# Leaky activation of a fused attention, MLP and switch-MoE kernel: slope and bend on ScalarE, and the rounding handed from GpSimd to ScalarE two tiles later

## Chip, cores and metric

One core of one Trainium2 chip runs the whole program. The time is device microseconds of one execution; for each kernel the median of several executions is taken. The profile is of one further execution.

## What is computed

Top-32 attention (4 batches, 8 heads, 576 tokens, width 64), then an MLP with a leaky activation, then a mixture of 8 experts. The change touches the second:

```
x = attention output as 2304 rows of 512
h = x @ w_in                                  # 512 -> 2048
g = maximum(h, 0) + alpha * minimum(h, 0)     # alpha: one value for each of the 2048 columns
x2 = g @ w_out                                # 2048 -> 512, all float32
```

## The kernel before

**Attention.** There are 16 passes. A pass takes four heads and half of the 576 query rows, as nine tiles of 128 rows, in three groups of three tiles; group 0, 1 and 2 below. For each group VectorE searches the 32nd largest score of every row (`search`: MAX8 at L1050 and MATCH_REPLACE8 at L1063 in four rounds), then masks and sums the exponentials (L1070). The reciprocal of the sums (`invert`: L1079 and L1082) is computed inside the search of the following group, after its first two MAX8. GpSimd multiplies the three tiles by it (`normalise`, L1324), TensorE transposes them (L560, L561), ScalarE copies the transposes out (L856, L857), and TensorE multiplies by v (L571). ScalarE also copies the scores (L835) and computes the exponentials (L841, L844). Pass p+1's scores for groups 0 and 1 are made between the transposes of pass p.

**MLP.** A step is two passes, an even and an odd one. There are 8 steps; in steps 1 to 7 the 288 tokens of the step before also go through the MLP, and the last 288 go through it in a tail behind the last step. x, w_in, w_out and g are each split into a high and a low float16 part, and each product is three float16 matmuls. During the even pass TensorE makes h for 16 tiles f of 128 columns (L590, `up`), between transposes and score matmuls; during the odd pass it makes x2 (L604, `down`). `up` has two PSUM banks: tile f waits until ScalarE has read tile f-2. `down` waits for all 16 tiles of g (`g_ready`).

**The leak, for each tile f.** ScalarE, in `mlp_part`: Relu with scale s to `pos_part` (L882), Relu with scale -s to `neg_part` (L883), and, after waiting for its own semaphore, `neg_part` times -alpha (L886). Then `leak` on GpSimd: the sum (L358), the float16 high part (L360, a TENSOR_SCALAR), and sum minus high part (L362, the low part), each waiting for the one before. In the tail VectorE runs the same `leak`. `pos_part` and `neg_part` have four buffers; ScalarE's tile f waits until the low part of tile f-4 is done.

**Order on each engine.** Each engine works through a written order, and nothing overtakes. GpSimd in the even pass of steps 1 to 7: normalise group 0, two `low_x` subtractions, leak of tiles 0 to 4; normalise group 1, leak of tiles 5 to 11; normalise group 2, leak of tiles 12 to 15; then normalise group 0 of the odd pass. ScalarE in the even pass: for group 0 and then group 1, and for each of the three tiles j: copy the transposes, one or two leak tiles, copy a score tile, one or two leak tiles; with j = 0 it ends with the exponentials of the next group. So tiles 0 and 1 stand before the exponentials of group 1, tiles 8 and 9 before those of group 2, and tiles 14 and 15 are the last thing in the even pass. The odd pass begins on TensorE and ScalarE with group 2's transposes (the tiles of the even pass), score matmuls between them, and the products with v.

**Weights.** In step 0, without an MLP, ScalarE scales each of eight chunks of 2048 columns (four of w_in, then four of w_out) in place (L932) and rounds it (L936), and GpSimd subtracts (`split`). VectorE works out the scales in `close_weights` and `scale_weights` with small linked instructions between its searches.

```
leak_parts = {(0, 0): range(0, 5), (0, 1): range(5, 12), (0, 2): range(12, FT1)}
normalise(2 * i + par, par, g)
if g == 0:
    low_x(2 * i + par - 1)
leak(pool, nc.gpsimd, i - MLP_LAG, leak_parts.get((par, g), ()))
```

## Time and profile before

| | before |
|---|---|
| median of 3 runs | 1118.12 us (1116.74 to 1120.65) |
| profiled execution | 1123.2 us, span 1121.4 us |
| busy: TensorE, VectorE | 927.9 us (83%), 903.8 us (81%) |
| busy: ScalarE, GpSimd | 631.4 us (56%), 427.4 us (38%) |
| mean granted TensorE clock | 0.934 of full speed |

In the profile PE is TensorE's matmuls and PEld its weight loads, DVE is VectorE, ACT ScalarE, POOL GpSimd. L358 is line 358 of the kernel before. Times are microseconds from the start of the span unless marked ns. Behind an instruction, square brackets give how long its engine sat idle before it and who ended that.

### The profile page before, as it was taken

How to read it: one execution, taken by the hardware profiler on the slowest of the kernel's cores; microseconds unless marked ns; L12 is line 12 of the kernel's file. 1: busy time of each engine (PE TensorE's matmuls, PEld its weight loads, DVE VectorE, ACT ScalarE, POOL GpSimd, SP SyncE). 2: the span in 40 equal slices, each digit the busy share in tenths (PEclk: the TensorE clock that was granted, in tenths of full speed). 3: DMA queues.
4: the chain of work that ended last, by engine and by line, in shares of the span. 5: the costliest groups of instructions: out<-in, count | busy, mean ns of one | idle time of the engine just before them, and what ended most of it. 6: DMA issues, size and time to landing. Idle time of an engine off the chain costs nothing.

```text
span 1121.4 us, 22533 instructions
## 1 busy us (share of the span) xinstructions
PE 927.9 (83%) x6271; PEld 616.9 (55%) x6272; DVE 903.8 (81%) x1984; ACT 631.4 (56%) x1324; POOL 427.4 (38%) x598
## 2 busy tenths in 40 slices
PE   5346588898899889888988898899888889498996
PEld 2223256675666657665766575667556567243342
DVE  4999989999999999999999999999999270611110
ACT  3786969647855785587459637954883281010100
POOL 0136738514830682267028513840582100201110
PEclk9956589999999999999999999999999799699999
DMA  7910110013002200310031004001100166626650
GB/s 205 365 37 22 32 34 22 23 41 87 0 21 70 57 0 21 96 32 21 1 97 30 21 8 119 1 21 53 44 2 1 55 226 213 221 90 225 199 165 18
DMA packets 98658, 84.05 MB, mean 75 GB/s; under 512 B 69116, under 2 KB 77308, under 8 KB 98048
## 3 DMA queue, kind: packets, MB, share of 16 engines
q1 hardware_dynamic: 94544, 78.56, 23.0%
q0 software_dynamic: 1488, 3.15, 0.8%
q10 hardware_dynamic: 2528, 1.18, 0.4%
q8 instruction: 43, 0.70, 0.3%
q14 instruction: 55, 0.45, 0.1%
HBM read 72.64 MB, written 11.53 MB: 75 GB/s over the span
## 4 chain that ended last, share of the span: by engine, by line
PE 62%; POOL 12%; issue 11%; ACT 8%; DVE 4%; DMA 2%; POOLq 1%; ACTq 0%; DVEq 0%
PE acc L604 16%; PE acc L571 8%; PE sc L542 7%; PE pt_full L560 6%; PE acc L590 5%; POOL pos_part L358 5%; PE sc L712 3%; PE pt_full L772 3%; POOL arena L360 3%; POOL arena L1324 2%; PE pt_full L780 2%; PE sc L721 2%; PE acc L613 2%; ACT arena L844 1%; PE acc L619 1%
## 5 line engine op out<-in xcount | busy, mean ns | idle before, releaser
L1050 DVE MAX8 best<-arena 128x8 f32<-128x576 f32 x576 | 403.5, 742 | 9.8 <-ACT arena L835 6.6
L1063 DVE MATCH_REPLACE8 arena<-best,arena 128x576 f32<-128x576 f32 x432 | 315.8, 738 | 0.0
L1324 POOL TENSOR_SCALAR arena<-arena,row_inv 128x576 f32<-128x576 f32 x144 | 106.5, 757 | 351.3 <-DVE row_inv L1082 351.3
L590 PE MATMUL acc<-arena 128*128 (+1 forms) x1536 | 202.4, 286 | 28.0 <-ACT neg_part L883 26.1
L604 PE MATMUL acc<-arena 128*128 128x288 f16 x1536 | 202.2, 289 | 2.9 <-issue 2.9
L590 PEld LDWEIGHTS acc<-arena 128*128 128x128 f16 x1536 | 146.4, 98 | 78.8 <-issue 38.9
L604 PEld LDWEIGHTS acc<-arena 128*128 128x128 f16 x1536 | 149.6, 99 | 49.6 <-issue 12.9
L560 PE MATMUL pt_full<-ident,arena 128*128 128x128 f32 x576 | 102.4, 306 | 60.0 <-POOL arena L1324 34.4
L835 ACT ACTIVATE arena<-sc 128x576 f32<-128x576 f32 x144 | 92.1, 642 | 87.1 <-PE sc L542 70.6
L1070 DVE SCALAR_TENSOR_TENSOR arena<-arena,best 128x576 f32<-128x576 f32 x144 | 126.7, 927 | 5.9 <-ACT arena L844 5.9
L560 PEld LDWEIGHTS pt_full<-ident,arena 128*128 128x128 f32 x576 | 73.1, 155 | 90.3 <-POOL arena L1324 42.9
L542 PE MATMUL sc<-kT,qT 64*128 64x288 f32 x512 | 113.0, 478 | 7.0 <-ACT arena L835 5.0
L358 POOL TENSOR_TENSOR pos_part<-pos_part,neg_part 128x288 f32<-128x288 f32 x112 | 96.6, 863 | 48.6 <-ACT neg_part L886 48.6
L571 PE MATMUL acc<-arena,nat 128*64 128x288 f32 (+1 forms) x640 | 92.9, 431 | 20.4 <-ACT arena L857 13.7
L844 ACT ACTIVATE arena<-arena,neg_max 128x576 f32<-128x576 f32 x144 | 101.2, 765 | 1.6
L856 ACT ACTIVATE arena<-pt_full 128x512 f32<-128x512 f32 x128 | 75.5, 590 | 44.3 <-PE pt_rest L561 42.3
L362 POOL TENSOR_TENSOR arena<-pos_part,arena 128x288 f16<-128x288 f32 x112 | 86.7, 774 | 16.7 <-POOL arena L360 1.1
L542 PEld LDWEIGHTS sc<-kT,qT 64*128 64x128 f32 x512 | 63.1, 210 | 39.3 <-issue 20.1
L571 PEld LDWEIGHTS acc<-arena,nat 128*64 128x64 f32 (+1 forms) x640 | 45.0, 141 | 65.0 <-issue 49.8
L882 ACT ACTIVATE pos_part<-acc,scale 128x288 f32<-128x288 f32 x128 | 63.4, 495 | 26.6 <-PE acc L590 25.8
L886 ACT ACTIVATE neg_part<-neg_part,neg_alpha 128x288 f32<-128x288 f32 x128 | 68.5, 535 | 4.2
L883 ACT ACTIVATE neg_part<-acc,neg_scale_g 128x288 f32<-128x288 f32 x128 | 63.1, 493 | 0.0
(172 smaller groups left out, 942.2 us busy)
## 6 DMA issues: line engine op xcount, KB each, us to landing
arena<-in_moe_w_dram SPq DMA_DIRECT2D x64, 512.0 KB, 4.2
nat<-in_v_dram SPq DMA_DIRECT2D x64, 128.0 KB, 2.2
nat<-in_k_dram SPq DMA_DIRECT2D x60, 128.0 KB, 2.8
x_rows<-x2n SPq DMA_DIRECT2D x24, 192.0 KB, 2.4
out_dram<-x2n SPq DMA_DIRECT2D x24, 192.0 KB, 2.6
nat<-in_q_dram SPq DMA_DIRECT2D x64, 64.0 KB, 2.1
arena<-in_moe_w_in_dram SPq DMA_DIRECT2D x4, 1024.0 KB, 7.4
arena<-in_moe_w_out_dram SPq DMA_DIRECT2D x4, 1024.0 KB, 14.5
```

What stands on the lines that cost most here:

```text
L358: unit.tensor_tensor(pos, pos, neg, ALU.add).then_inc(leak_ready, 1)
L542: last = nc.tensor.matmul(dst[:, c, 0:HALF], qT[at, h // 2, r * P:(r + 1) * P], kT[at, h // 2, c * HALF:(c + 1) * HALF], start=True, stop= ...
L560: nc.tensor.transpose(pt_full[:, kt, :], src[:, kt * P:(kt + 1) * P], ident[:, :])
L571: last = nc.tensor.matmul(dst[h * D:(h + 1) * D, 0:HALF], v_nat[0:rows, par, 2 * c + h, kt, :], probsT[0:rows, 2 * c + h, kt, :], start=(k ...
L590: last = nc.tensor.matmul(dst[:, 0:HALF], win16[:, a, d, f * P:(f + 1) * P], xT16[:, bass.ds(row + d, 1), b, :].rearrange("p b s -> p (b s)"),
L604: last = nc.tensor.matmul(items.open[:, 0:HALF], wout16[:, a, f // (FT1 // OUT_CHUNKS), f % (FT1 // OUT_CHUNKS) * DM + d * P:f % (FT1 // O ...
L835: nc.scalar.activation(scores[:, t, :].rearrange("p (c s) -> p c s", c=2), sc[(TILES * par + t) % 2][:, :, 0:HALF], ACT.Copy).then_inc(s_s ...
L844: nc.scalar.activation(probs[:, gp, j, :], scores[:, GROUP * g + j, :], ACT.Exp, bias=neg_max[:, gp, j:j + 1], scale=SCALE).then_inc(exp_r ...
L1050: nc.vector.max(best[:, gp, j, r, :], src).then_inc(max_found if r == 0 else dve_step, 1)
L1063: nc.vector.match_replace(left[:, j, :], best[:, gp, j, r, :], src, MASKED).then_inc(dve_step, 1)
L1070: nc.vector.scalar_tensor_tensor(out=probs[:, gp, j, :], in0=tiles[j], scalar=best[:, gp, j, ROUNDS - 1, 7:8], in1=probs[:, gp, j, :], op0 ...
L1324: nc.gpsimd.tensor_scalar(probs[:, gp, j, :], probs[:, gp, j, :], row_inv[:, gp, j:j + 1], 1.0, ALU.mult, ALU.mult)\
```

## The change

ScalarE now reads h out of PSUM twice and no more: Copy with a scale `slope`, and Relu with a scale `bend`, both with one value for each column. slope is s times the smaller of alpha and 1, bend is s times (1 - alpha), and for alpha above 1 both signs are turned round by a `sign` that is also multiplied into w_out. GpSimd adds the two (`leak_sum`, waiting for `acc_stored`). The float16 high part is no longer GpSimd's: ScalarE rounds the sum of tile f-2 behind its two instructions for tile f (`round_leak`), and behind tile 15 the sums of 13, 14 and 15. GpSimd takes the low part of tile f-2 behind the sum of tile f (`leak_low`), and the last three behind sum 15. In the tail (the last 288 tokens) VectorE still adds, rounds and subtracts. In step 0 the scaling of a w_out chunk becomes four instructions of 512 columns instead of one of 2048, and VectorE has eight small instructions more and two less. No DMA is added, removed or moved.

```
-                        nc.scalar.activation(pos_part[:, f % NEG, :], src[:, 0:HALF], ACT.Relu, scale=scale[:, 3:4])
-                        nc.scalar.activation(neg_part[:, f % NEG, :], src[:, 0:HALF], ACT.Relu, scale=neg_scale_g[:, 0:1])\
+                        nc.scalar.activation(pos_part[:, f % NEG, :], src[:, 0:HALF], ACT.Copy, scale=slope[:, f:f + 1])
+                        nc.scalar.activation(neg_part[:, f % NEG, :], src[:, 0:HALF], ACT.Relu, scale=bend[:, f:f + 1])\
                             .then_inc(acc_stored, 1)
-                        act.wait_ge(acc_stored, items.base + items.used)
-                        nc.scalar.activation(neg_part[:, f % NEG, :], neg_part[:, f % NEG, :], ACT.Copy, scale=neg_alpha[:, f:f + 1])\
-                            .then_inc(parts_ready, 1)
+                        if not (isinstance(m, int) and m == HALVES - 1):
+                            for whole in range(f - 2, f - 1 if f < FT1 - 1 else FT1):
+                                if whole >= 0:
+                                    round_leak(m, whole)
...
+            def round_leak(m, f):
+                act.wait_ge(leak_summed, FT1 * m + f + 1)
+                nc.scalar.activation(gT16[0][:, f, :], pos_part[:, f % NEG, :], ACT.Copy).then_inc(leak_rounded, 1)
...
+        def leak_sum(engine, unit, m, first_item, f):
+            hold(engine, acc_stored, first_item + f + 1)
+            unit.tensor_tensor(pos_part[:, f % NEG, :], pos_part[:, f % NEG, :], neg_part[:, f % NEG, :], ALU.add).then_inc(leak_summed, 1)
+
+        def leak_low(engine, unit, m, f):
+            hold(engine, leak_rounded, FT1 * m + f + 1)
+            unit.tensor_tensor(gT16[1][:, f, :], pos_part[:, f % NEG, :], gT16[0][:, f, :], ALU.subtract).then_inc(g_ready, 1)
...
-                        leak(pool, nc.gpsimd, i - MLP_LAG, leak_parts.get((par, g), ()))
+                        for f in leak_parts.get((par, g), ()):
+                            leak_sum(pool, nc.gpsimd, i - MLP_LAG, LOOP_BASE + (i - MLP_LAG) * FULL_ITEMS + PV_ITEMS + PREP_ITEMS, f)
+                            for low in range(f - 2, f - 1 if f < FT1 - 1 else FT1):
+                                if low >= 0:
+                                    leak_low(pool, nc.gpsimd, i - MLP_LAG, low)
...
-                    nc.scalar.activation(raw[:, n, :], raw[:, n, :], ACT.Copy, scale=scale[:, k:k + 1]).then_inc(w_scaled, 1)
+                        for f in range((n - DT) * FT1 // OUT_CHUNKS, (n - DT + 1) * FT1 // OUT_CHUNKS):
+                            at = slice(f % (FT1 // OUT_CHUNKS) * DM, (f % (FT1 // OUT_CHUNKS) + 1) * DM)
+                            last = nc.scalar.activation(raw[:, n, at], raw[:, n, at], ACT.Copy, scale=sign[:, f:f + 1])
...
-                nc.vector.tensor_scalar(neg_alpha[:, :], alpha_sb[:, :], -1.0, None, ALU.mult)
+                link_scale(nc.vector.tensor_scalar(slope[:, :], alpha_sb[:, :], 1.0, None, ALU.min))
+                link_scale(nc.vector.tensor_scalar(sign[:, :], alpha_sb[:, :], 1.0, -2.0, ALU.is_gt, ALU.mult))
+                link_scale(nc.vector.tensor_scalar(sign[:, :], sign[:, :], 1.0, None, ALU.add))
+                link_scale(nc.vector.tensor_tensor(slope[:, :], slope[:, :], sign[:, :], ALU.mult))
+                link_scale(nc.vector.tensor_scalar(bend[:, :], alpha_sb[:, :], -1.0, 1.0, ALU.mult, ALU.add))
...
-                scale_of(1, 3).then_inc(scale_ready, 1)
+                link_scale(scale_of(1, 3))
+                nc.vector.tensor_scalar(sign[:, :], sign[:, :], scale[:, 2:3], None, ALU.mult).then_inc(scale_ready, 1)
...
-                nc.vector.tensor_scalar(neg_scale_g[:, :], scale[:, 3:4], -1.0, None, ALU.mult)
+                nc.vector.tensor_scalar(slope[:, :], slope[:, :], scale[:, 3:4], None, ALU.mult)
+                nc.vector.tensor_scalar(bend[:, :], bend[:, :], scale[:, 3:4], None, ALU.mult)
```

## Rows read from the trace of the kernel before

**Rows 1.** The page, busy time, share of the span and instructions of each engine.
```profile
PE 927.9 (83%) x6271; PEld 616.9 (55%) x6272; DVE 903.8 (81%) x1984; ACT 631.4 (56%) x1324; POOL 427.4 (38%) x598
```
**Rows 2.** Busy time in one step of 106 us (count), then clock and DMA.
```profile
260.00:366.00 106.00, 95.00 (x722) 67.42 (x718) 104.61 (x229) 70.30 (x152) 49.12 (x70) 0.98 0.15 39
```
**Rows 3.** VectorE in order of time, steps 2 and 3 (start, length).
```profile
277.30 0.15 DVE L1082 RECIPROCAL row_inv<-row_den 128x3 f32<-128x3 f32 x1
...
296.19 0.15 DVE L1082 RECIPROCAL row_inv<-row_den 128x3 f32<-128x3 f32 x1
...
314.50 0.15 DVE L1082 RECIPROCAL row_inv<-row_den 128x3 f32<-128x3 f32 x1
...
331.31 0.15 DVE L1082 RECIPROCAL row_inv<-row_den 128x3 f32<-128x3 f32 x1
...
347.86 0.76 DVE L1050 MAX8 best<-arena 128x8 f32<-128x576 f32 x1 [1.06 <-issue]
```
**Rows 4.** The chain that ended last, 360 to 470 us, merged (start, length, what).
```profile
388.41 2.21 POOL arena L1324 x3
...
407.45 0.76 POOL arena L1324
```
**Rows 5.** GpSimd in order of time, even pass of step 2.
```profile
280.28 0.80 POOL L358 TENSOR_TENSOR pos_part<-pos_part,neg_part 128x288 f32<-128x288 f32 x1
281.24 0.43 POOL L360 TENSOR_SCALAR arena<-pos_part 128x288 f16<-128x288 f32 x1 [0.16 <-POOL pos_part L358]
281.82 0.73 POOL L362 TENSOR_TENSOR arena<-pos_part,arena 128x288 f16<-128x288 f32 x1
282.54 2.20 POOL L1324 TENSOR_SCALAR arena<-arena,row_inv 128x576 f32<-128x576 f32 x3
```
**Rows 6.** TensorE in order of time, steps 2 and 7.
```profile
302.40 0.66 PE L560 MATMUL pt_full<-ident,arena 128*128 128x128 f32 x4 [0.84 <-POOL arena L1324]
...
844.40 0.98 PE L560 MATMUL pt_full<-ident,arena 128*128 128x128 f32 x4 [2.13 <-POOL arena L1324]
```
**Rows 7.** ScalarE in order of time, even pass of step 2 and what follows.
```profile
289.81 0.19 ACT L841 ACTIVATE neg_max<-best 128x3 f32<-128x3 f32 x1
...
292.68 0.49 ACT L882 ACTIVATE pos_part<-acc,scale 128x288 f32<-128x288 f32 x1
293.06 0.49 ACT L883 ACTIVATE neg_part<-acc,neg_scale_g 128x288 f32<-128x288 f32 x1
293.58 0.54 ACT L886 ACTIVATE neg_part<-neg_part,neg_alpha 128x288 f32<-128x288 f32 x1
294.03 0.48 ACT L882 ACTIVATE pos_part<-acc,scale 128x288 f32<-128x288 f32 x1
...
303.20 0.60 ACT L856 ACTIVATE arena<-pt_full 128x512 f32<-128x512 f32 x1
```
**Rows 8.** ScalarE's groups by line and shape: busy us, mean ns, idle before.
```profile
L932 ACT ACTIVATE arena<-arena,scale 128x2048 f32<-128x2048 f32 x8 | 15.9, 1990 | 0.0
...
L873 ACT ACTIVATE arena<-x 128x288 f32 x24 | 10.6, 444 | 4.2 <-ACT x L871 4.2
```
**Rows 9.** The chain that ended last in step 0, 60 to 180 us.
```profile
113.29 1.90 ACT arena L932
...
120.00 1.90 ACT arena L932
```
**Rows 10.** VectorE in step 0.
```profile
150.46 0.82 DVE L1070 SCALAR_TENSOR_TENSOR arena<-arena,best 128x576 f32<-128x576 f32 x1 [3.37 <-ACT arena L844]
```
**Rows 11.** All engines in order of time, tail, end of `up`.
```profile
920.78 0.49 ACT L883 ACTIVATE neg_part<-acc,neg_scale_g 128x288 f32<-128x288 f32 x1
...
921.87 0.46 DVE L358 TENSOR_TENSOR pos_part<-pos_part,neg_part 128x288 f32<-128x288 f32 x1 [0.17 <-ACT neg_part L886]
```
**Rows 12.** Busy time, clock and DMA in two stretches (6 and 2 us).
```profile
290.00:296.00 6.00, 4.11 (x35) 3.21 (x34) 5.67 (x10) 5.91 (x13) 5.24 (x7) 1.00 0.00 0
...
846.00:848.00 2.00, 2.00 (x10) 1.23 (x9) 2.00 (x4) 1.97 (x6) 1.19 (x2) 0.50 0.00 0
```

More of the change, by code:

```diff
@@ L169, in topk_attention_prelu_mlp_switch_moe @@
         unscale = sb("unscale", [P, 4])
-        neg_scale_g = sb("neg_scale_g", [P, 1])
         x2_scale = sb("x2_scale", [P, 1])
-        neg_alpha = sb("neg_alpha", [P, FT1])
+        slope = sb("slope", [P, FT1])
+        bend = sb("bend", [P, FT1])
+        sign = sb("sign", [P, FT1])
         x32 = sb("x32", [P, 2, HALF])
@@ L283, in topk_attention_prelu_mlp_switch_moe @@
         x2_written = sem("x2_written")
-        parts_ready = sem("parts_ready")
-        leak_ready = sem("leak_ready")
+        leak_summed = sem("leak_summed")
+        leak_rounded = sem("leak_rounded")
         g_ready = sem("g_ready")
@@ L349, in topk_attention_prelu_mlp_switch_moe @@
         assert PARTS % DT == 0
-        LEAK_STEPS = 2
-        def leak(engine, unit, m, fs):
-            for f in fs:
-                n = LEAK_STEPS * (FT1 * m + f)
-                pos, neg = pos_part[:, f % NEG, :], neg_part[:, f % NEG, :]
-                hold(engine, parts_ready, FT1 * m + f + 1)
-                unit.tensor_tensor(pos, pos, neg, ALU.add).then_inc(leak_ready, 1)
-                hold(engine, leak_ready, n + 1)
-                unit.tensor_scalar(gT16[0][:, f, :], pos, 1.0, 1.0, ALU.mult, ALU.mult).then_inc(leak_ready, 1)
-                hold(engine, leak_ready, n + 2)
-                unit.tensor_tensor(gT16[1][:, f, :], pos, gT16[0][:, f, :], ALU.subtract).then_inc(g_ready, 1)
+        def leak_sum(engine, unit, m, first_item, f):
[4 more added lines that the diff above has]
+            unit.tensor_tensor(gT16[1][:, f, :], pos_part[:, f % NEG, :], gT16[0][:, f, :], ALU.subtract).then_inc(g_ready, 1)
         def load_stage(engine, n):
@@ L928, in high_weights @@
                 for n in split_slots.get(GROUPS * (2 * i + par) + g, ())[half:half + 1] if isinstance(i, int) and i < MLP_LAG else ():
-                    k = 1 if n < DT else 2
                     act.wait_ge(scale_ready, 1)
                     act.wait_ge(raw_loaded[n], 16)
-                    nc.scalar.activation(raw[:, n, :], raw[:, n, :], ACT.Copy, scale=scale[:, k:k + 1]).then_inc(w_scaled, 1)
+                    if n < DT:
+                        last = nc.scalar.activation(raw[:, n, :], raw[:, n, :], ACT.Copy, scale=scale[:, 1:2])
+                    else:
+                        for f in range((n - DT) * FT1 // OUT_CHUNKS, (n - DT + 1) * FT1 // OUT_CHUNKS):
+                            at = slice(f % (FT1 // OUT_CHUNKS) * DM, (f % (FT1 // OUT_CHUNKS) + 1) * DM)
+                            last = nc.scalar.activation(raw[:, n, at], raw[:, n, at], ACT.Copy, scale=sign[:, f:f + 1])
+                    last.then_inc(w_scaled, 1)
                     act.wait_ge(w_scaled, n + 1)
@@ L1162, in _ @@
             for m in range(HALVES - MLP_LAG, HALVES):
-                leak(dve, nc.vector, m, range(FT1))
+                for f in range(FT1):
+                    leak_sum(dve, nc.vector, m, TAIL_BASE + PV_ITEMS, f)
+                    dve.wait_ge(leak_summed, FT1 * m + f + 1)
+                    nc.vector.tensor_scalar(gT16[0][:, f, :], pos_part[:, f % NEG, :], 1.0, 1.0, ALU.mult, ALU.mult).then_inc(leak_rounded, 1)
+                    leak_low(dve, nc.vector, m, f)
             def link(ins):
```

## The prediction

> **What bounds the kernel now.** I read the page first: no engine is full over the span, TensorE 83%, VectorE 81% [rows 1]. The busy time by step says more: in each 106 us of steps 1 to 6 VectorE works 104.6 us and TensorE 95.0 [rows 2]. That looks like a VectorE bound. The order of time says it is only half so. From one reciprocal to the next VectorE needs 16.81 us when nothing disturbs it (314.50 to 331.31), but 18.89 to 296.19 and 18.31 to 314.50, and before the next step's first group it stands 1.06 us for a score tile [rows 3]. Six undisturbed groups are 100.9 us and a step takes 105.9 (the normalisation of group 1 at 282.54 and at 388.41 [rows 4, 5]), so about 5 us of a step are not VectorE's own work. What the others wait for is in the chain that ended last: in every even pass it goes through GpSimd's leak tiles and enters TensorE by its normalisations of group 1 (388.41) and group 2 (407.45) [rows 4]. GpSimd works off tiles 2 to 15 without a pause: a tile costs 0.80 + 0.43 + 0.73 us with two waits for itself, 2.26 us from 280.28 to 282.54, and only then does it normalise group 1, whose reciprocal had been there since 277.30 [rows 3, 5]. TensorE waits 0.84 us for the same at group 2 [rows 6]. So the loop is bound by a chain of TensorE and ScalarE in written order, with GpSimd's leak inside it, and VectorE runs just behind.
>
> **The change, part by part.** I follow one step, in the times of step 2.
>
> *GpSimd.* A leak tile becomes a sum and a low part, no longer waiting for itself: 0.80 + 0.73 less an overlap of 0.04 each, 1.45 us instead of 2.26 [rows 5], 0.8 us less for each of 16 tiles. Group 1 is normalised some 3 us earlier and no longer holds TensorE.
>
> *ScalarE.* The third instruction of a tile costs 0.52 to start behind L883 (293.06 to 293.58, it waits for its own semaphore) and 0.45 more to the next one, where two unlinked ones are 0.38 apart [rows 7]. The rounding has neither that wait nor a scale operand; its like is L873, 0.44 us against 0.54 [rows 7, 8], so 0.39 to the next. That saves 0.19 us for each tile. Tiles 0 and 1 have no rounding behind them, so the exponentials of group 1 begin 0.14 + 0.45 = 0.6 us earlier. With the wait for group 1 gone (0.3 us) and 0.2 us of savings on tiles that TensorE does not pace, the exponentials of group 2 start 1.1 us before 289.81, and tile 10's second instruction ends at 292.5 instead of 293.55 [rows 7].
>
> *The new wait.* From there GpSimd is serial again: sum 10, low 8, sum 11, low 9 (2.9 us), the three normalisations of group 2 (2.20), then sums 12 to 15 with lows 10 to 12 between them (4 x 0.76 + 3 x 0.69, 5.2 us): sum 15 is there at 292.6 + 10.3 = 302.9 [rows 5]. Group 2's reciprocal doesn't delay this: VectorE loses less to GpSimd here and gives it near 294.6, GpSimd comes at 295.5. ScalarE has finished tile 15 at about 301.6, rounds 13 and 14, waits for sum 15, rounds it to 303.3, and only then copies group 2's first transposes: 303.3, against 303.20 before [rows 7]. Queued behind the waiting rounding are those copies, the score copies, the next exponentials; TensorE's second transpose waits for the first copy. So nearly 2 us that TensorE has gained by then (its transposes of group 2 can begin at 300.5, not 302.40 [rows 6]) are given back. What stays: TensorE makes the first score tile in that pause, which ScalarE waited for before. I take 0.35 us a step as kept. Six steps end with that handover: -2.0 us. Bounds: 1.2 us a step kept if rounding 15 were ready at once, 0.4 lost if a sum and low pair took 1.65 us, nearer to what they are when VectorE disturbs them.
>
> *VectorE.* In the odd group that ends at 314.50 it loses 1.5 us to GpSimd's leak (18.31 against 16.81 [rows 3]). GpSimd will be done by then. In steps 1 to 6 this only becomes a longer wait for scores, 1.06 us growing to over 2. In step 7, with no scores behind it, TensorE waits 2.13 us for that reciprocal [rows 6]; there it counts: -1.3 us (0 to 2).
>
> Here a rule of the Trainium skill speaks for more. By "SBUF — State Buffer", section "Who interferes with whom", a VectorE instruction with two SBUF inputs contends with a GpSimd instruction that reads SBUF. The trace agrees in that the reciprocals are late where leak tiles run [rows 3]. That would price the change by GpSimd's shorter occupancy; it is the third rival below.
>
> *Step 0.* L932 takes 1990 ns for 2048 columns, L886's form 540 ns for 288 [rows 7, 8]; between them 512 columns cost 0.72 us, 0.63 with the overlap of 0.09. Four are 2.5 us against 1.90: +0.6 for each chunk. Chunks 4 and 5 stand in the chain at 113.29 and 120.00 [rows 9]; the rounding of chunk 7 is level with it, chunk 6 has some slack. Three count: +1.9 us (nothing if the split costs no more than its columns, 2.6 if all count and overlap less). The Trainium skill, "ScalarE: Activation LUTs", section "What ACT_TABLE_LOAD costs", states for a [128,1] scale operand an ACTIVATE of about 280 ns + 0.833 ns a column with 93 ns of overlap; an estimate by that page is 4 x 0.61 = 2.45 us, which would make this term +1.7. VectorE's six more small instructions cost some 0.2 us each (a small one takes 0.15 [rows 3], and most wait for the one before), 1.1 us; they are hidden by the 3.37 us that it waits for exponentials at 150.46 [rows 10]. Without that cover they'd cost that 1.1.
>
> *Tail.* The last tile's chain loses L886: VectorE's sum started 1.09 us after L883 began (920.78 to 921.87) [rows 11]; it can start after 0.53. -0.55 us, as `down` waits for it. The other 15 tiles run under TensorE's matmuls.
>
> Sum: 1.9 - 2.0 - 1.3 - 0.55 = -2.0 us. The profiled execution took 1123.2 us (span 1121.4), 5 us above the median of the runs, 1118.12. I apply the difference to the median: 1116.
>
> **The rivals.**
> *The gain is kept.* If ScalarE got sum 15 as soon as it is ready for it, the even pass would keep nearly 2 us: six steps give -11.7, with the rest -11.7 + 1.9 - 1.9 = -12, 1106 us. For it: the chain names GpSimd twice a step [rows 4]. Against: group 2's 2.20 us of normalisation and tiles 12 to 15 stand before that sum in GpSimd's order.
> *Slower by the new wait.* If GpSimd's pair costs 1.65 us or more instead of 1.45, sum 15 comes 1.4 us later. From 0.35 us on, a step loses. That is about +1.0 a step, +6, with the rest +6 to 1124. For it: every GpSimd instruction has a wait on a register here. Against: L362 starts its successor 0.72 us on with such a wait [rows 5].
> *VectorE relieved.* If VectorE is the true bound, a step falls by what GpSimd takes from it, 1.5 in the one group and about 1.2 of 2.08 in the other [rows 3], 2.7 us, seven times: -19, 1101 with the step 0 cost. Against: it already waits for scores.
> *The clock.* TensorE gets a new pause of about 1.6 us before the second transpose of group 2. Behind the 2.13 us pause of step 7 the granted clock was 0.50 for a while, 1.2 GHz, while in 290 to 296, where TensorE stands 1.89 of 6 us, it stayed 1.00, 2.4 GHz [rows 6, 12]. If it falls in each step, transposes and scores there take 1.6 us more: 6 x 1.6 - 2 = +8, 1126.
> That the change does not do what it says has little room: the instructions are counted in the code.
>
> **How the numbers follow.** Within 0.3% is 3.35 us either way, about what a measurement of this kernel tells from no change. My case 0.55, with its own range 1112 to 1120; gain kept in full or large part 0.17; VectorE relieved 0.05; slower by the wait 0.14; clock 0.09. Of my case 0.08 lies below 1114.8. Faster 0.30, same 0.50 (my case's 0.47 and weak forms of the slower ones), slower 0.20. The range reaches halfway into both sides, 1107 to 1122.
>
> **What would show it.** L360 gone from GpSimd but for the 16 of the tail on VectorE; the wait for L1324 before TensorE's transposes of group 2 gone, and in its place ScalarE idle before the last rounding of each half, ended by GpSimd's sum, with TensorE waiting for ScalarE's L857 behind it. The reciprocals' spacing in the odd group down from 18.3 to 16.8, and VectorE's wait for scores up from 1.1 to over 2 us. Step length 105.4. ScalarE's w_out scaling at 2.5 us. I am wrong if a step gets shorter by more than 1 us, or if ScalarE stands for GpSimd at other tiles than the last.

## The result, and the profile after

The kernel after takes 1144.62 us (median of 4, 1141.9 to 1145.68) against 1119.24 (median of 4) for the kernel before on the same chip: ratio 1.023, 95% interval 1.0207 to 1.0253. It is 25 us slower, where 2 us faster was forecast. Its profiled execution took 1145.68 us (span 1143.9).

The page, busy time of each engine, answers to [rows 1]:

```profile
PE 943.9 (83%) x6271; PEld 623.6 (55%) x6272; DVE 897.6 (78%) x1990; ACT 603.0 (53%) x1320; POOL 368.0 (32%) x486
```

and the window of one step of the loop to [rows 2]:

```profile
366.00:475.25 109.25, 97.14 (x720) 68.20 (x718) 103.53 (x229) 67.11 (x152) 40.67 (x54) 0.95 0.14 38
```

Every unit but TensorE works less, as the change promised: GpSimd 59 us, ScalarE 28 us, VectorE 6 us. TensorE has the same 6271 matmuls and is busy 16 us longer, and the granted clock of the step is 0.95 instead of 0.98.

Three stretches add up to the difference of the spans, 22.5 us: up to the first reciprocal of step 1 (154.09 before, 156.27 after) +2.2; from there to the last one of the loop (875.81, 900.55) +22.6; behind it -2.2. Forecast were +1.9, -3.3 and -0.55. So the error is in the loop. The waits of TensorE by releaser (total us, times, longest) say where, first before, then after:

```profile
PE pt_full L560 <- POOL arena L1324: 34.4, 19, 10.6
...
PE pt_full L560 <- ACT arena L857: 17.2, 9, 5.3
```

```profile
PE pt_full L556 <- ACT arena L853: 39.1, 16, 5.4
PE pt_full L556 <- POOL arena L1340: 26.0, 4, 10.6
```

The wait for GpSimd in front of the transposes has become rare (19 times became 4, with the longest, 10.6 us, in both), and the wait for ScalarE's copies has taken its place. I look at one such place, the start of the odd pass of step 3, where group 2's normalised tiles are transposed. In what follows it is called the odd head; the even head is the start of the next even pass, behind the router's matmuls (L609, L615). Tile 0 of `up` begins at 380.40 here; in the steps of [rows 6, 7] it began at 265.48. GpSimd first, then ScalarE, then TensorE and two rows of VectorE, each in order of time. L354 is the sum and L358 the low part on GpSimd; on ScalarE L882 is the first instruction of a tile, L874 a rounding, L852 and L853 the copy of a transpose; on TensorE L556 are transposes, L538 scores, L567 the products with v:

```profile
407.29 1.12 POOL L354 TENSOR_TENSOR pos_part<-pos_part,neg_part 128x288 f32<-128x288 f32 x1 [2.49 <-ACT neg_part L883]
408.37 1.25 POOL L358 TENSOR_TENSOR arena<-pos_part,arena 128x288 f16<-128x288 f32 x1
...
411.31 2.19 POOL L1340 TENSOR_SCALAR arena<-arena,row_inv 128x576 f32<-128x576 f32 x3 [0.24 <-DVE row_inv L1088]
413.46 0.80 POOL L354 TENSOR_TENSOR pos_part<-pos_part,neg_part 128x288 f32<-128x288 f32 x1
414.21 0.74 POOL L358 TENSOR_TENSOR arena<-pos_part,arena 128x288 f16<-128x288 f32 x1
...
417.79 0.79 POOL L354 TENSOR_TENSOR pos_part<-pos_part,neg_part 128x288 f32<-128x288 f32 x1
```

```profile
414.98 0.50 ACT L882 ACTIVATE pos_part<-acc,slope 128x288 f32<-128x288 f32 x1 [1.83 <-POOL arena L358]
...
416.42 0.50 ACT L882 ACTIVATE pos_part<-acc,slope 128x288 f32<-128x288 f32 x1 [0.22 <-POOL arena L358]
...
418.61 0.44 ACT L874 ACTIVATE arena<-pos_part 128x288 f16<-128x288 f32 x1 [0.63 <-POOL pos_part L354]
418.96 0.58 ACT L852 ACTIVATE arena<-pt_full 128x512 f32<-128x512 f32 x1
```

```profile
414.99 0.60 PE L556 MATMUL pt_full<-ident,arena 128*128 128x128 f32 x4
...
415.63 1.23 PE L538 MATMUL sc<-kT,qT 64*128 64x288 f32 x4
419.84 1.09 PE L556 MATMUL pt_full<-ident,arena 128*128 128x128 f32 x4 [2.98 <-ACT arena L853]
...
421.07 2.29 PE L538 MATMUL sc<-kT,qT 64*128 64x288 f32 x8
...
425.75 7.33 PE L567 MATMUL acc<-arena,nat 128*64 128x288 f32 x40 [1.13 <-ACT arena L853]
...
407.68 1.34 DVE L1076 SCALAR_TENSOR_TENSOR arena<-arena,best 128x576 f32<-128x576 f32 x1
...
426.95 0.82 DVE L1076 SCALAR_TENSOR_TENSOR arena<-arena,best 128x576 f32<-128x576 f32 x1 [2.69 <-ACT arena L840]
```

The reader is to see four things. The sum of tile 10 and the low part of tile 8 (407.29, 408.37) take 1.12 and 1.25 us where an undisturbed pair takes 0.80 and 0.73; VectorE's L1076 at 407.68 takes 1.34 us beside them instead of 0.81, and that puts all that follows on GpSimd some 0.8 us back. Then GpSimd takes the low part of tile 10 only at 414.21, behind the three normalisations, and ScalarE's tile 14, which needs tile 10's buffers, waits 1.83 us for that: a wait that I had not listed. Then the last rounding waits 0.63 us for sum 15, and the copy starts at 418.96. TensorE, which had made its first transposes at 414.99 and the scores behind them, pauses 2.98 us for it. And from the second transpose on every matmul takes longer than in an undisturbed place: 1.09 us against 0.60 for the same four transposes, and 7.33 us for the products with v, where the kernel before has:

```profile
308.23 5.52 PE L571 MATMUL acc<-arena,nat 128*64 128x288 f32 x40 [1.13 <-ACT arena L857]
```

The windows of the same stretch (PE, PEld, DVE, ACT, POOL busy, then the granted clock) show why:

```profile
416.00:418.00 2.00, 0.86 (x4) 0.35 (x2) 2.00 (x5) 1.76 (x5) 2.00 (x4) 1.00 0.00 0
418.00:420.00 2.00, 0.16 (x1) 0.19 (x2) 2.00 (x4) 1.39 (x4) 2.00 (x4) 0.80 0.00 0
420.00:422.00 2.00, 2.00 (x9) 1.48 (x10) 2.00 (x7) 0.98 (x3) 0.64 (x1) 0.50 0.00 0
...
426.00:428.00 2.00, 2.00 (x10) 1.11 (x10) 1.05 (x3) 1.97 (x4) 0.00 (x0) 0.50 0.00 0
428.00:430.00 2.00, 2.00 (x12) 0.73 (x8) 2.00 (x7) 0.18 (x1) 0.00 (x0) 0.64 0.00 0
430.00:432.00 2.00, 2.00 (x18) 1.06 (x16) 2.00 (x5) 0.94 (x2) 1.09 (x2) 1.00 0.00 0
```

The clock is at 0.50 (1.2 GHz) from 420 to 428. It fell at this place in every step from 2 to 7. The reciprocals answer to [rows 3] (odd pass of step 2):

```profile
301.75 0.15 DVE L1088 RECIPROCAL row_inv<-row_den 128x3 f32<-128x3 f32 x1
...
321.35 0.16 DVE L1088 RECIPROCAL row_inv<-row_den 128x3 f32<-128x3 f32 x1
...
338.16 0.15 DVE L1088 RECIPROCAL row_inv<-row_den 128x3 f32<-128x3 f32 x1
```

The group at the odd head takes 19.60 us (18.31 before, 16.81 forecast). The six gaps of a step are 17.97, 17.97, 19.60, 16.81, 17.96, 18.93 = 109.24 us; before, they were 17.09, 18.89, 18.29, 16.81, 17.96, 16.81 = 105.85.

The terms outside the loop came out nearly as forecast. The scaling of a w_out chunk, ScalarE's line in step 0, and the tail's sum on VectorE:

```profile
113.90 2.54 ACT L937 ACTIVATE arena<-arena,sign 128x512 f32<-128x512 f32 x4
...
946.72 0.46 DVE L354 TENSOR_TENSOR pos_part<-pos_part,neg_part 128x288 f32<-128x288 f32 x1 [0.17 <-ACT neg_part L883]
```

The 2.54 us run from the start of the first to the end of the last of the four, where the one instruction of the kernel before takes 1.99: 0.55 us more a chunk, against 0.6 forecast. The sum starts 0.53 us after ScalarE's L883 (946.19), as forecast.

### The profile page after: what moved, and what is told of

The parts are those of the page before. It is cut to its first block, busy times and chain, and to the rows that moved or that the text cites. A ratio compares the mean times of both kernels' runs of the same rounds, so it can differ in the third digit from the quotient of the medians.

```text
span 1143.9 us, 22199 instructions
## 1 busy us (share of the span) xinstructions
PE 943.9 (83%) x6271; PEld 623.6 (55%) x6272; DVE 897.6 (78%) x1990; ACT 603.0 (53%) x1320; POOL 368.0 (32%) x486
## 4 chain that ended last, share of the span: by engine, by line
PE 56%; issue 15%; DVE 10%; ACT 9%; POOL 4%; DMA 3%; SPq 2%; DVEq 1%; ACTq 0%; POOLq 0%
PE acc L600 16%; PE acc L586 6%; PE sc L538 6%; PE acc L567 5%; PE pt_full L556 5%; PE pt_full L768 3%; PE sc L708 3%; DVE arena L1076 3%; DVE best L1056 2%; DVE arena L1069 2%; PE pt_full L776 2%; PE sc L717 2%; PE acc L609 2%; ACT arena L840 1%; POOL pos_part L354 1%
## 5 line engine op out<-in xcount | busy, mean ns | idle before, releaser
L556 PE MATMUL pt_full<-ident,arena 128*128 128x128 f32 x576 | 103.1, 308 | 73.8 <-ACT arena L853 39.1
L1076 DVE SCALAR_TENSOR_TENSOR arena<-arena,best 128x576 f32<-128x576 f32 x144 | 119.3, 877 | 37.5 <-ACT arena L840 37.3
L556 PEld LDWEIGHTS pt_full<-ident,arena 128*128 128x128 f32 x576 | 74.1, 156 | 103.5 <-issue 60.9
L538 PE MATMUL sc<-kT,qT 64*128 64x288 f32 x512 | 119.3, 511 | 5.8 <-ACT arena L831 4.8
L567 PE MATMUL acc<-arena,nat 128*64 128x288 f32 (+1 forms) x640 | 103.8, 471 | 21.0 <-ACT arena L853 13.8
L354 POOL TENSOR_TENSOR pos_part<-pos_part,neg_part 128x288 f32<-128x288 f32 x112 | 92.0, 821 | 89.4 <-ACT neg_part L883 89.4
L852 ACT ACTIVATE arena<-pt_full 128x512 f32<-128x512 f32 x128 | 75.6, 591 | 48.9 <-PE pt_rest L557 47.9
L882 ACT ACTIVATE pos_part<-acc,slope 128x288 f32<-128x288 f32 x128 | 63.7, 498 | 60.7 <-PE acc L586 35.3
L567 PEld LDWEIGHTS acc<-arena,nat 128*64 128x64 f32 (+1 forms) x640 | 48.8, 154 | 73.4 <-issue 60.6
L358 POOL TENSOR_TENSOR arena<-pos_part,arena 128x288 f16<-128x288 f32 x112 | 87.7, 789 | 0.0
L538 PEld LDWEIGHTS sc<-kT,qT 64*128 64x128 f32 x512 | 65.2, 225 | 39.8 <-issue 19.3
L883 ACT ACTIVATE neg_part<-acc,bend 128x288 f32<-128x288 f32 x128 | 63.3, 494 | 0.0
L1293 DVE SCALAR_TENSOR_TENSOR nat<-pt_full,slot_gate,nat 128x512 f32<-128x512 f32 x8 | 6.0, 751 | 64.8 <-PE pt_full L768 36.3
```

The lines of the kernel that those rows point to most:

```text
L354: unit.tensor_tensor(pos_part[:, f % NEG, :], pos_part[:, f % NEG, :], neg_part[:, f % NEG, :], ALU.add).then_inc(leak_summed, 1)
L538: last = nc.tensor.matmul(dst[:, c, 0:HALF], qT[at, h // 2, r * P:(r + 1) * P], kT[at, h // 2, c * HALF:(c + 1) * HALF], start=True, stop= ...
L556: nc.tensor.transpose(pt_full[:, kt, :], src[:, kt * P:(kt + 1) * P], ident[:, :])
L567: last = nc.tensor.matmul(dst[h * D:(h + 1) * D, 0:HALF], v_nat[0:rows, par, 2 * c + h, kt, :], probsT[0:rows, 2 * c + h, kt, :], start=(k ...
L1076: nc.vector.scalar_tensor_tensor(out=probs[:, gp, j, :], in0=tiles[j], scalar=best[:, gp, j, ROUNDS - 1, 7:8], in1=probs[:, gp, j, :], op0 ...
```

## Experiments

The table gives for each kernel its ratio to the kernel before, and of its profiled execution the first reciprocal of step 1, the lengths of six steps (from the reciprocal at one odd head, 314.50 in [rows 3], to that at the next), and the half-rate time in each of them: the sum of (1 - clock) x 2 x 2 us over windows of 2 us, and where it lies. 3.4 us at half rate means 1.7 us of clock lost. The steps come from one profiled execution of each kernel, the median from all its executions, and the ratio is against the kernel before as measured on the same chip. Each experiment carries, ahead of its result, what was expected.

| kernel | median us | ratio (95%) | step 1 at | steps, us | half-rate time a step, us |
|---|---|---|---|---|---|
| before | 1119.24 | | 154.09 | 105.45 to 105.93 | 3.4, even head |
| after | 1144.62 | 1.023 (1.0207, 1.0253) | 156.27 | 109.23 to 110.23 | 10.2, odd head; first 17.1, last 13.7 |
| e1 | 1142.06 | 1.0212 (1.0191, 1.0233) | 155.65 | 108.90 to 109.24 | 10.2, even head |
| e2 | 1123.03 | 1.0028 (1.0007, 1.0049) | 157.21 | 104.91 to 106.56 | none to 6.8; 13.6 in the first, 13.7 in the last |
| e4 | 1128.85 | 1.0102 (1.0077, 1.0127) | 157.16 | 105.19 to 106.79, and 3 of 109 | 3.4 to 6.8; 13.6 in the long ones |
| e5 | 1150.27 | 1.0294 (1.0252, 1.0335) | 152.78 | 109.30 to 113.18 | 6.8, odd head, in three of 109.3; 10.2 to 13.7 in the others |
| e7 | 1152.91 | 1.0299 (1.0246, 1.0352) | 156.87 | 112.21 to 112.92, last 105.72 | 6.8, even head; last none |
| e8 | 1123.95 | 1.005 (1.0028, 1.0072) | 153.27 | 105.63 to 105.87 | none |
| e3b | 1119.55 | 0.999 (0.9957, 1.0023) | 152.90 | 103.53 to 106.01, one 109.0 | none to 13.6 |
| e9 | 1118.32 | 0.9984 (0.9957, 1.001) | 154.27 | 103.34 to 105.99 | none, one 3.4 |
| e10 | 1125.56 | 1.0062 (1.0039, 1.0086) | 156.51 | 105.25 to 105.47, first 107.14 | none, first 3.4 |
| e11 | 1140.72 | 1.0177 (1.0142, 1.0211) | 157.26 | 107.22 to 109.26 | 10.2, one 3.4 |
| e12 | 1151.23 | 1.028 (1.0254, 1.0307) | 153.32 | 106.74 to 114.92 | none to 13.6 |
| e6 | 1139.60 | 1.0186 (1.0169, 1.0204) | 154.44 | 106.86 to 110.23 | 10.2, odd head; first 3.4, second 17.1, last 13.6 |
| e13 | 1126.98 | 1.0056 (1.0023, 1.0088) | 152.61 | 105.72 to 105.86 | none |
| e14 | 1135.76 | 1.0132 (1.0092, 1.0173) | 152.42 | 106.75 to 106.86, one 112.0 | none, 13.7 in that one |
| e15 | 1130.57 | 1.0085 (1.0047, 1.0122) | 155.10 | 104.20 to 105.27, two of 112 | none to 3.4; 10.2 in the long ones |

**e1: fill the pause at the odd head.** The kernel after, with matmuls whose result nobody reads.

```
+ if mlp and par and j == 0:          # odd head, behind the first scores
+     hold(pe, acc_stored, items.base + items.used)
+     for _ in range(18):
+         nc.tensor.matmul(acc[0][:, 0:HALF], win16[:, 0, 0, 0:P], win16[:, 0, 0, 0:HALF], start=True, stop=True)
```

> The changed kernel with 18 matmuls of 288 float16 columns, whose product nobody reads, in the pause of TensorE that follows group 2's first transposes and score matmuls at the head of the odd pass. ScalarE's wait for sum 15 is untouched. Theory (the pause of 3.0 us lets TensorE's clock fall to 0.50 for about 9 us, and that is most of the loss): granted clock stays 1.00 there, the products with v take 5.5 us again and not 7.3, a step is 105.3 to 106.2 us instead of 109.3, median about 1120 us. Rival (the late copies alone cost the time, the clock has little to do with it): step above 107.5 us, median above 1132 us.

The clock stayed at 1.00 at the odd head and its group went from 19.60 to 17.42 us. But the step stayed at 109.23: the half-rate stretch had moved to the even head, whose group went from 18.93 to 21.09. The windows there:

```profile
464.00:466.00 2.00, 1.32 (x17) 1.33 (x16) 2.00 (x5) 0.50 (x1) 0.78 (x2) 1.00 0.00 0
466.00:468.00 2.00, 2.00 (x15) 1.97 (x15) 2.00 (x6) 0.19 (x1) 0.00 (x0) 0.55 0.02 4
...
474.00:476.00 2.00, 2.00 (x10) 1.34 (x10) 1.56 (x3) 0.84 (x3) 0.00 (x0) 0.50 0.57 131
```

and VectorE, which in that head waits for exponentials of scores that came late:

```profile
479.74 0.82 DVE L1080 SCALAR_TENSOR_TENSOR arena<-arena,best 128x576 f32<-128x576 f32 x1 [4.18 <-ACT arena L844]
```

So filling the pause keeps the clock up at the odd head, but the theory that this fall alone makes the loss was wrong: either a fall elsewhere costs as much, or something else holds the step at 109.2.

**e2: undo the queueing.** The kernel after with the last three roundings moved behind the odd head's copies and exponentials.

```
-                            for whole in range(f - 2, f - 1 if f < FT1 - 1 else FT1):
-                                if whole >= 0:
-                                    round_leak(m, whole)
+                            if 2 <= f < FT1 - 1:
+                                round_leak(m, f - 2)
...
  exps(p, par, 0)
+ if par:
+     for whole in range(FT1 - 3, FT1):
+         round_leak(i - MLP_LAG, whole)
```

> The changed kernel with the last three roundings of each half (tiles 13, 14 and 15) moved on ScalarE from the end of the even pass to behind group 2's copies and the exponentials of the odd pass's group 0. Theory (copies queued behind the wait for sum 15 start the loss): TensorE's pause falls to about 1.3 us, the clock stays up, step 103.8 to 105 us, median about 1109 us. Rival (the other waits of ScalarE for GpSimd, ahead of tile 14 above all, are what counts): step above 107 us, median above 1130 us.

```profile
412.81 0.63 PE L556 MATMUL pt_full<-ident,arena 128*128 128x128 f32 x4 [1.30 <-ACT arena L853]
```

TensorE's pause fell from 2.98 to 1.30 us, and nearly all of the loss went: 1.0028. Tile 14 still waited 1.83 us for tile 10. The three roundings in front of the copies are what makes the long pause; this is shown. The gain that was expected on top (steps of 103.8 to 105, a median of 1109) did not come: the steps are 105.8 us on average, no shorter than before. Its first and last step have 13.6 and 13.7 us at half rate and take only 106.06 and 105.50 us, no longer than its steps with 3.4 us (106.56, 106.52): so half-rate time has no fixed price.

**e11: undo the other wait.** The kernel after, with tiles 12 and 13 summed, and 10 and 11 lowered, before group 2 is normalised.

```
-leak_parts = {(0, 0): range(0, 5), (0, 1): range(5, 12), (0, 2): range(12, FT1)}
+leak_parts = {(0, 0): range(0, 5), (0, 1): range(5, 14), (0, 2): range(14, FT1)}
```

> The kernel after with one edit: leak tiles 12 and 13 are lowered before GpSimd's normalisation of group 2 instead of behind it; the last three roundings stay where they are. Theory (the roundings queued before the copies make the loss; tile 14's wait of 1.83 us ends before the sums of 14 and 15 do): copies of group 2 within 0.5 us of the kernel after, TensorE's pause 2.0 to 3.0 us, steps 108.5 to 109.3, median 1138 to 1145 (1.017 to 1.023). Rival (tile 14's wait is the cause): pause under 1.5 us, steps 105 to 106.5, median 1118 to 1125.

ScalarE in order of time, then TensorE:

```profile
307.25 0.44 ACT L874 ACTIVATE arena<-pos_part 128x288 f16<-128x288 f32 x1 [0.99 <-POOL pos_part L354]
```

```profile
308.48 1.09 PE L556 MATMUL pt_full<-ident,arena 128*128 128x128 f32 x4 [2.79 <-ACT arena L853]
```

Tile 14 no longer waits for GpSimd (it waits 0.58 us for TensorE instead), but the last rounding now waits 0.99 us for its sum instead of 0.63, and the pause is 2.79 us. 1.0177 is a little below the kernel after, inside what was expected. In its last three steps the clock fell for 3.4 us at the odd head behind pauses of 2.8 us and for 6.8 us at the even head. Tile 14's wait, missing in my working, is a defect of it but not the cause: it ends in a wait for sums 14 and 15 that comes in any case.

**e5: only the delay, in the kernel before.** Eight small ScalarE instructions in front of the odd head's copies.

```
+ if j == 0 and mlp and par:
+     for n in range(8):
+         at = slice(n % 2 * HALF // 2, (n % 2 + 1) * HALF // 2)
+         nc.scalar.activation(x2T[:, n // 2, at], ident[:, 0:1].to_broadcast([P, HALF // 2]), ACT.Copy, scale=alpha_sb[:, 0:1])
```

> The kernel before with eight small ScalarE instructions (144 columns each, about 2.5 us in all, written to a tile that is overwritten later) ahead of group 2's copies at the head of each odd pass with an MLP. Theory (a pause there costs its length and then the clock): granted clock falls to 0.50 behind it, step 110 us or more, median 1145 to 1155 us. Rival (a late copy costs only its own length or less): step at most 108.3 us, median at most 1137 us, clock 1.00.

```profile
422.70 0.63 PE L560 MATMUL pt_full<-ident,arena 128*128 128x128 f32 x4 [2.08 <-ACT arena L857]
```

A pause of 2.0 to 2.1 us in the kernel before, with nothing of the change in it, makes every step longer. Three steps take 109.3 us with the half-rate time at the odd head; the other three take 109.9 to 113.2 us, with falls at the even head too, and in one of them a pause of 2.06 us brought no fall at the odd head. The loss is reproduced, and somewhat more (1.0294).

**e4: slope and bend alone.** The kernel after, with GpSimd rounding as before and ScalarE rounding nothing.

```
-                            for whole in range(f - 2, f - 1 if f < FT1 - 1 else FT1):
-                                if whole >= 0:
-                                    round_leak(m, whole)
...
+ hold(pool, leak_summed, FT1 * (i - MLP_LAG) + f + 1)
+ nc.gpsimd.tensor_scalar(gT16[0][:, f, :], pos_part[:, f % NEG, :], 1.0, 1.0, ALU.mult, ALU.mult).then_inc(leak_rounded, 1)
+ leak_low(pool, nc.gpsimd, i - MLP_LAG, f)
```

> Slope and bend alone: ScalarE has two instructions for a tile and no rounding, GpSimd adds, rounds and subtracts as in the kernel before; w_out is scaled in four pieces. Theory (the loss comes with the rounding on ScalarE): step about 105.2 us, median 1116 to 1119 us. Rival (the two instructions with a scale for each column, or the pieces in step 0, carry the loss): median above 1130 us.

1.0102, a half loss, between the theory (up to 1119 us) and the rival (over 1130 us): three steps of 105.2 to 106.8 us and three of 108.8 to 109.2. All have their half-rate time at the even head, 3.4 to 6.8 us in the short ones and 13.6 in the long ones. So the same code runs at both lengths, depending on how long the clock is down, and here without any rounding on ScalarE.

**e7 and e8: fill the even head as well.** e7 is e1 with 14 unused matmuls around the router's; e8 has those 14 alone, in the kernel before.

```
+ hold(pe, acc_stored, items.base + items.used - 1)
+ fill(bank, 5)                       # the same unused matmul, 5 times
...
  dst = begin(items, after_last=True)
  for j in range(NJ):
+     fill(1 - bank, 3)
```

> The kernel of the first fill run (18 unused matmuls at the head of the odd pass) with 14 more such matmuls around the 24 nine-column matmuls of the router in steps 1 to 6 and 7, where the fall of the clock went in that run: 5 in the wait ahead of them, 3 ahead of each of the three groups. The tail has none. Theory, revised (the half-rate time, wherever it falls, makes the loss of the changed kernel, since TensorE's own chain sets the step): the granted clock is 1.00 through the steps, a step is 105 to 106.3 us instead of 109.2, median 1115 to 1124 us. Rival (the clock has little to do with it and ScalarE's waits set 109.2): step 109 us or more, median 1140 to 1150 us.

> The kernel before with the same 14 unused matmuls around the router's nine-column matmuls in each step, where its clock is at 0.50 for 3.4 us in every step. Theory: the clock stays at 1.00, which gives back about 1.7 us of a step and costs 1.2 us for the matmuls: step 105.0 to 105.6 us, median 1113 to 1118 us. Rival (this fall lies in slack that VectorE leaves, so only the matmuls' cost shows): step 106 to 107 us, median 1120 to 1128 us.

e8 held the clock at 1.00 through these steps, and they stayed at 105.7 us: the 3.4 us of half rate in the kernel before lie in slack. Its median, 1124 us, is in the rival's range. e7 answers nothing about the clock, because something else came in. In five of its six steps TensorE stood 3.1 to 3.8 us (here 3.08) in front of the even head's transposes with no engine to wait for ("issue"), and the queue that loads instructions had 90 packets against 43 in the kernels before and after. TensorE in order of time, and the page's row of that queue (packets, MB, share):

```profile
367.87 0.65 PE L556 MATMUL pt_full<-ident,arena 128*128 128x128 f32 x4 [3.08 <-issue]
```

```profile
q8 instruction: 90, 1.47, 0.6%
```

I read this as TensorE waiting for its own instructions where the loop turns. That reading is argued from the profile, not tested by itself; more rows for it stand in the last section.

**e10 and e13: both heads filled, with fewer matmuls.** 9 in the odd head, and 5 + 1 for each text tile round the router; e10 in the kernel after, e13 in the kernel before.

> The kernel after, with 9 unused matmuls (128x288) after the first scores of the next pass's group 3 and with 5 + one per text tile of them around the router's matmuls: half of the first fill and a third of the second, so that TensorE need not wait for its own instructions where the loop turns. Theory (the steps of 109.2 us are the price of the half-rate stretch, wherever it falls among the two heads): with 3.4 us of half-rate time or less in a step the steps are 105.0 to 106.2 us, the median 1118 to 1124 (0.998 to 1.004 of before). Rival (the later copies and MAX8 waits set the step, the clock only fills slack): steps stay 109.2, median 1140 to 1144 (1.019 to 1.023), with the clock at 1.00 in both heads. If a stretch of 10 us at half rate is left in either head, the run says only that it costs 3.4 again.

> The kernel before with the same unused matmuls as the filled kernel after (9 in the odd head, 5 + one per text tile around the router). Its odd head had no stretch at half rate and its even head's lay in slack (filling it alone gave 1.005), so if the fills are free: steps 105.4 to 105.9 us, median 1118 to 1125 (0.999 to 1.005), and the filled kernel after stands at 1.001 to 1.006 of it. Rival (the clock at half rate did cost the kernel before): steps under 105.2, median under 1116.

e10 settles the rival that e1 had left. The window of one step of it, then TensorE's second transpose at the odd head and VectorE's row behind it:

```profile
366.00:471.45 105.45, 95.18 (x738) 67.78 (x735) 103.47 (x229) 67.08 (x154) 40.87 (x54) 1.00 0.15 40
```

```profile
413.97 0.63 PE L556 MATMUL pt_full<-ident,arena 128*128 128x128 f32 x4 [1.13 <-ACT arena L868]
...
418.90 0.82 DVE L1091 SCALAR_TENSOR_TENSOR arena<-arena,best 128x576 f32<-128x576 f32 x1 [0.52 <-ACT arena L855]
```

All waits of the change are still there (the copy at 413.09 came behind a rounding that waited 0.64 us), but the clock is at 1.00 and the step takes 105.45 us. 109.24 - 105.45 = 3.8 us a step are the clock's: 2.2 in the group at the odd head (19.60 to 17.44) and 1.6 in the one at the next even head (18.93 to 17.3), which TensorE reaches late. e13 is the control: 105.79 us a step on average. So with the clock held, the change makes a step 0.34 us shorter. (e10's first step, with 3.4 us at half rate, took 107.14 and is left out.) The two ratios, 1.0062 and 1.0056, differ by 0.0006, with the intervals combined 0.004 either way: no difference in the whole time. Why the fills cost some 0.5% of the median in both, while the loop in e13's profile is not longer (875.99 against 875.81 at its last reciprocal), stays open; part of it is that the profiled execution of before (1123.2) lies above its median and that of e13 (1124.62) below its own. Both medians came out 1 to 2 us above what was expected, the steps as expected.

**e12 and e14: the delay with fills.** e5 with the 18 matmuls of e1, and e5 with both small fills.

> The kernel before with both the eight small ScalarE instructions that put off the copies of group 2 by some 2.5 us (which alone gave 1.0294, steps 109.3) and the 18 unused matmuls that fill TensorE's pause there. If the delay costs by the clock of the odd head alone: that head at 1.00, steps 106 to 107.5, median 1122 to 1132 (1.003 to 1.011). If the fall only moves to the even head, as it did in the filled kernel after: steps 109 to 110, median 1142 to 1152 (1.020 to 1.029).

> The kernel before with the delay of some 2.5 us on ScalarE and both fills. If the delay costs by the clock alone: no stretch at half rate in the heads, steps 105.4 to 106.5 us, median 1119 to 1128 (1.000 to 1.008), against 1.029 for the delay alone. Rival (the late exps and copies hold VectorE whatever the clock): steps 107.5 to 109.5, median 1135 to 1150.

e12 went in the main as e1 had. Its steps vary: those of 106.7 and 107.0 us have no half-rate time, those of 109.4 and 112.1 have 6.8 and 13.6 us of it at the even head. In the longest, 114.92, TensorE also stood 4.62 us at the loop's turn with no engine to wait for, as in e7. e14 parts the delay from the clock. Five of its steps take 106.8 us, 1.0 more than e13: that is the delay by itself. The remaining 2.5 of the 3.5 us that e5's three steps of 109.3 lose are the clock's. In the fifth of the six the clock fell for 13.7 us, and that step took 112.0. Both rivals of the expectation had a part, the clock the larger one.

**e6: the split scaling.** w_out scaled in one instruction a chunk, without the per-tile sign.

> The kernel after with w_out scaled in one instruction a tile, as before (the leak's weights with one scale; the output is then wrong in sign for the tiles where sign is negative, times and shapes are the same). Theory: the split costs what the extra ScalarE instructions take in step 0, so the reciprocal at the start of step 1 comes at 153.5 to 155 instead of 156.27, the steps stay 109.2, median 1140 to 1143 (0.997 to 0.9985 of after). Rival: step 0's extra time is in the loads, not in ScalarE: start of step 1 stays at 156 to 157, median 1143 to 1146.

Step 1 began at 154.44 and the median was 1139.6, just below what was expected. (For slopes up to 1, as in these inputs, the sign is 1 and nothing of the output is lost.) Over all runs: with the code of before step 1 begins at 153.1 on average (6 kernels, 152.42 to 154.09), with the change at 156.7 (7 kernels, 155.65 to 157.26), with the change but whole chunks at 154.2 (4 kernels, 152.90 to 155.10). The change costs step 0 about 3.6 us, the split 2.5 of them, with a scatter of some 1 us either way from kernel to kernel.

**e3b, e9 and e15: a version without the losses.** e3b joins e2, e11 and e6; e9 adds e8's fill, e15 both small fills.

> The same as the run before it in this list but without the matmuls around the router. Theory (the clock falls there for 3.4 us or more in a step, as in the kernel before): step 104 to 105.8 us, median 1104 to 1116 us. Rival: as there, above 1116 us.

> The run with the deferred roundings, and further: GpSimd normalises group 2 behind tile 13 instead of behind tile 11, w_out is scaled in one piece for each chunk (with the sign left out, which is 1 for these inputs), and the 14 unused matmuls stand around the router's. Theory: ScalarE no longer waits at tile 14, TensorE never pauses long, clock 1.00, step 103.5 to 104.8 us, step 0 back to within 1 us of the kernel before, median 1100 to 1110 us. Rival (what was gained at GpSimd is not on the chain): step 105.5 us or more, median above 1116 us.

> The kernel after with the last three roundings behind the copies and exps, tiles 12 and 13 lowered before the normalisation of group 2, w_out scaled in one instruction a tile, and both small fills. If what the filled kernel after still loses is the queueing on ScalarE and step 0: start of step 1 at 153 to 154.5, steps 104.8 to 105.4, median 1114 to 1119 (0.996 to 1.000). Rival (the loss is in the fills or the tail): as the filled kernel after, 1122 to 1127 (1.003 to 1.007).

e3b and e9 are level with the kernel before (0.999, 0.9984, both intervals hold 1), where 1104 to 1116 and 1100 to 1110 us had been expected: above 1116, as their rivals said. e15 missed both of its ranges. Its four undisturbed steps take 104.8 us on average, 1.0 less than e13's, but twice TensorE stood over 5 us at the loop's turn, and the clock fell for 10.2 us (TensorE in order of time, then the page's row of the queue):

```profile
253.36 1.11 PE L556 MATMUL pt_full<-ident,arena 128*128 128x128 f32 x4 [5.24 <-issue]
```

```profile
q8 instruction: 63, 1.03, 0.4%
```

No version beat the kernel before by more than a measurement tells.

## Why the prediction was wrong

**The step that failed is the clock.** I listed it as a rival, priced 1.6 us a step and given 0.09. The place was right, the second transpose of group 2. Its price was 3.8 us a step, for two reasons. I priced only transposes and scores; but in the rows above the products with v take 7.33 us instead of 5.52 too. And I took the delay at the odd head for the whole of it, while 1.6 us are added in the next even head. Its condition was also taken too lightly: the pause was forecast at 1.6 us and came out at 2.98 (the copies came 0.75 us late, TensorE was there 0.4 us early), and I had weighed one fall behind 2.13 us [rows 6] against one stretch without a fall, and chose the latter. The Trainium skill, "TensorE: Matmul & The Clock Gate", section "HAM oscillation — how this bites in real kernels", tells of a loop in which TensorE's wait (there for a DMA) brings the clock down anew in each turn; this case's trace agrees in kind (0.50 at the odd head of every step from 2 to 7, for step 3 in the windows above), though in e5 one pause of 2.06 us brought no fall.

**The handover** ("nearly 2 us that TensorE has gained by then are given back"; "I take 0.35 us a step as kept"). Qualitatively it held: GpSimd's wait at group 2 went, TensorE was there 34.6 us after tile 0 (forecast 35.0, before 36.9), and its gain ended in a wait for ScalarE's copies. The copies came 38.56 us after tile 0, against 37.8 forecast: GpSimd began group 2's normalisation at 30.9 instead of 30.0, because the first pair ahead of it took 2.3 us beside VectorE's L1076 instead of 1.45 (the rows at 407.29 to 408.37); the pairs behind it took 1.44 us each as forecast. I also missed tile 14's wait for low part 10, ScalarE standing for GpSimd at another tile than the last, which the prediction had named as a sign of being wrong; e11 shows that it changes little. With the clock held, the step is 0.34 us shorter (105.79 to 105.45), which is the 0.35 of the forecast. So close an agreement is luck: sum 15 came 0.75 us late, and by the forecast's own measure ("From 0.35 us on, a step loses") the step should have lost.

**Last step's VectorE** (-1.3) did not show: the group there took 19.73 us (18.29 before), as TensorE paused 1.96 us and the clock fell there as well. In e10 it took 17.44: 0.85 us of the 1.3.

**Step 0** (+1.9): 2.2 in the two profiles, 3.6 on the averages over kernels. One chunk costs 2.54 us against 1.99, 0.55 more where 0.6 was forecast. The estimate by the Trainium skill ("ScalarE: Activation LUTs", section "What ACT_TABLE_LOAD costs"), 2.45 us against 1.90, gives the same 0.55, and the trace agrees: the four instructions start 0.61 us apart. e6 gives 2.5 us for the split on the averages and 1.8 between its profile and that of the kernel after, so whether three chunks count (1.65 us) or all four (2.2) can't be told. About 1 us more is from other parts of the change; which, no run tells.

**Tail** (-0.55): the sum starts 0.53 us after L883, as forecast. The stretch behind the last reciprocal is 2.2 us shorter in the profiles; it also has some 3 us less of half-rate time, so how much of the 2.2 is the forecast term is not shown.

**The sum** therefore: in four of the six steps 3.8 us of clock less 0.34, +3.4 each; the first and the last lost 4.3 and 4.2; that is 22.2 of the loop's 22.6. Step 0 +2.2, tail -2.2.

**Still open:** why so many kernels (after, e1, e4, e5, e6, e11) have steps of 108.8 to 109.3 us, whether 6.8, 10.2 or 13.6 us of a step are at half rate; why the same time costs nearly nothing in e2; and what decides between a fall of 3.4 and of 10 us. How short the odd head's pause must be was not measured beyond this: pauses of 2.9 to 3.1 us (after) brought 10.2 us at half rate into the odd head in five steps and 3.4 in one, 1.96 us in its last step brought 6.8, 2.7 to 2.9 us (e11) brought 3.4 or 10.2, 2.0 to 2.1 us (e5) mostly 6.8 and once none, 1.2 to 1.5 us (e2) none to 6.8.

## What to carry to other kernels

When work is moved to an engine that also feeds TensorE, look at what is queued behind the moved instruction where it has to wait, and sum up TensorE's pause there; if the trace of before has one fall of the clock behind a pause of like length, price the fall for every turn of the loop, with all matmuls that follow and the delay that they hand on, and say that it costs less where TensorE has slack. To learn what the clock costs, hold it up with unused matmuls and compare with a control that has the same filling; filling one pause only may move the fall. Defer work that nobody needs soon behind the instructions that others wait for.

## What the hardware showed that was not expected

The half-rate stretch can move as a whole: filled at one head, it turned up at the other with the same 10.2 us (e1), where TensorE had no pause over 0.7 us but ran the router's 24 matmuls of 9 columns. And a few unused matmuls more in the loop brought pauses of 3.1 to 5.3 us at its turn that no engine caused: five in e7 (32 matmuls more), two in e15 (17), one in e12 (18); none in e1 (18), e10, e13 and e14 (17). The packets on the instruction queue go with the pauses, nine for each: 45 in the four kernels without one, 54 in e12, 63 in e15, 90 in e7. Why kernels with the same number of matmuls differ stays open.
